# Second MLP: the polynomial's product q(q - 2.5) on ScalarE and GpSimd instead of VectorE

## The reference

```python
def _moe2_ref(x, w_in, w_out) -> np.ndarray:
    h = x @ w_in
    g = h - np.tanh(h)
    return (g @ w_out).astype(np.float32)
```

## Time and profile before

| | |
|---|---|
| median of 3 runs | 1000.71 us (999.56 to 1003.57) |
| span of the profiled execution | 998.4 us |
| TensorE matmuls busy | 971.2 us, 97% |
| VectorE busy | 647.0 us, 65% |
| GpSimd busy | 405.3 us, 41% |
| ScalarE busy | 389.3 us, 39% |
| mean granted TensorE clock | 0.998 of full speed |

### The profile page before, as it was taken

One profiled execution on the slowest core, in us unless ns is written; L12 is line 12 of the kernel. 1 busy time (PEld: TensorE's weight loads), 2 busy tenths in 40 slices (PEclk: granted clock), 3 DMA queues, 4 the chain that ended last, 5 costly groups with the idle time before them and its releaser, 6 DMA issues.

```text
span 998.4 us, 17710 instructions
## 1 busy us (share of the span) xinstructions
PE 971.2 (97%) x6120; PEld 947.5 (95%) x6120; DVE 647.0 (65%) x1136; ACT 389.3 (39%) x790; POOL 405.3 (41%) x398
## 2 busy tenths in 40 slices
PE   8899999999999999999999999999999999999997
PEld 7799999999999999999999889999999999999997
DVE  5954444444444444444446679998999889998886
ACT  4321211211221212112113366665666566666654
POOL 5754453443544444435434553332333233333332
PEclk9999999999999999999999999999999999999999
DMA  8511112021111111120121300000000000000000
GB/s 235 137 25 25 25 25 48 3 48 25 24 25 26 25 24 25 24 48 2 25 83 45 127 1 1 25 1 25 0 24 0 25 0 17 7 9 17 9 17 25
DMA packets 86251, 32.43 MB, mean 32 GB/s; under 512 B 75937, under 2 KB 83106, under 8 KB 86178
## 3 DMA queue, kind: packets, MB, share of 16 engines
q1 hardware_dynamic: 86178, 31.47, 12.3%
HBM read 26.74 MB, written 4.72 MB: 32 GB/s over the span
## 4 chain that ended last, share of the span: by engine, by line
PE 50%; issue 39%; POOL 6%; DVE 2%; POOLq 0%; ACT 0%; DVEq 0%; ACTq 0%
PE bank L634 13%; PE bank L636 12%; PE bank L635 12%; PE bank L709 4%; POOL g_l L409 4%; PE bank L692 2%; PE bank L705 2%; PE bank L701 2%; POOL wout_l L367 1%; PE bank L673 1%; PE bank L679 1%; POOL g_l L359 1%; PE bank L715 1%; DVE win_l L922 1%; POOL wout_l L417 0%
## 5 line engine op out<-in xcount | busy, mean ns | idle before, releaser
L634 PE MATMUL bank<-x_h,win_h 128*128 128x384 f32 x768 | 258.0, 336 | 7.4 <-DVE g_f L910 4.5
L636 PE MATMUL bank<-x_h,win_l 128*128 128x384 f32 x768 | 257.6, 335 | 0.0
L635 PE MATMUL bank<-x_l,win_h 128*128 128x384 f32 x768 | 257.2, 335 | 0.0
L409 POOL TENSOR_TENSOR g_l<-g_f,g_h 128x384 fp32r<-128x384 f32 x128 | 129.9, 1015 | 280.9 <-ACT g_h L513 280.9
L475 ACT ACTIVATE g_h<-g_f 128x384 fp32r<-128x384 f32 x128 | 67.2, 525 | 425.7 <-DVE g_f L910 425.7
L359 POOL TENSOR_TENSOR g_l<-g_f,g_h 128x384 fp32r<-128x384 f32 x128 | 132.0, 1032 | 245.9 <-ACT g_h L475 238.7
L908 DVE TENSOR_SCALAR g_f<-bank 128x384 f32<-128x384 f32 x128 | 71.3, 557 | 201.3 <-PE bank L636 199.3
L634 PEld LDWEIGHTS bank<-x_h,win_h 128*128 128x128 f32 x768 | 144.6, 188 | 9.4 <-DVE g_f L910 6.4
L635 PEld LDWEIGHTS bank<-x_l,win_h 128*128 128x128 f32 x768 | 144.7, 188 | 0.0
L636 PEld LDWEIGHTS bank<-x_h,win_l 128*128 128x128 f32 x768 | 144.7, 188 | 0.0
L967 DVE SCALAR_TENSOR_TENSOR area<-area 128x384 f32<-128x384 f32 x128 | 121.9, 952 | 35.1 <-ACT area L494 32.6
(11 more groups left out here) (99 smaller groups left out, 1396.7 us busy)
## 6 DMA issues: line engine op xcount, KB each, us to landing
out<-area SPq DMA_DIRECT2D x24, 192.0 KB, 1.9
x2T<-in_r SPq DMA_DIRECT2D x23, 192.0 KB, 2.8
x2T<-in_k SPq DMA_DIRECT2D x23, 192.0 KB, 3.4
x2T<-in_v SPq DMA_DIRECT2D x23, 192.0 KB, 3.5
x2T<-in_moe_w_in SPq DMA_DIRECT2D x4, 768.0 KB, 6.5
x2T<-in_moe_w_out SPq DMA_DIRECT2D x4, 768.0 KB, 6.0
area<-in_moe_w_in SPq DMA_DIRECT2D x4, 768.0 KB, 4.3
area<-in_moe_w_out SPq DMA_DIRECT2D x4, 768.0 KB, 4.5
```

The lines of the kernel that those rows point to most:

```text
L409: pool.tensor_tensor(g_l[:, m0 % 4, :], g_f[:, m0 % 2, :], g_h[:, m0 % 4, :].bitcast(F32), ALU.subtract).then_inc(s_gl2, 1)
L634: pe.matmul(dst, wh, xh, start=first, stop=False)
L635: pe.matmul(dst, wh, xl, start=False, stop=False)
L636: return pe.matmul(dst, wl, xh, start=False, stop=last)
```

## The change

ScalarE makes q - 2.5 (new function shifted), GpSimd multiplies it by q (new function square_poly), and VectorE's poly is gone. The compare takes poly's place in VectorE's step; it has moved from ahead of the product of m0 - 1 to behind it, and belongs to slot m0 now. On ScalarE make_ratio moves to the end of the step, behind hi2 of the slot before. On GpSimd square_poly of slot m0 + 1 stands ahead of lo2 of slot m0. The new semaphore s_qq goes from ScalarE to GpSimd; s_pp is now given by GpSimd.

```diff
+            def square_poly(b, m0):
+                m = SLOTS * b + m0
+                pool.wait_ge(s_qq, m + 1)
+                pool.tensor_tensor(ratio[m0 % 2], ratio[m0 % 2], sq[m0 % 2], ALU.mult).then_inc(s_pp, 1)
+
             PEELED = Q
+            square_poly(0, 0)
             for m0 in range(PEELED):
+                square_poly(0, m0 + 1)
                 lo2(0, m0)
...
             with pool.Fori(0, BODIES - 1) as b:
                 for n in range(SLOTS):
+                    square_poly(b, n + PEELED + 1)
                     lo2(b, n + PEELED)
             for n in range(SLOTS - PEELED):
+                if n + PEELED + 1 < SLOTS:
+                    square_poly(LAST, n + PEELED + 1)
                 lo2(LAST, n + PEELED)
...
+            def shifted(b, m0):
+                m = SLOTS * b + m0
+                act.wait_ge(s_sq, m + 1)
+                if is_due(m - 1):
+                    act.wait_ge(s_small, m - 1)
+                act.activation(ratio[m0 % 2], sq[m0 % 2], ACT.Copy, bias=C3_OVER_C5).then_inc(s_qq, 1)
...
                 if m0 < SLOTS or b is not LAST:
                     square(b, m0)
+                    shifted(b, m0)
                     if ends is not None:
                         keep_out(b, ends, 0)
-                    make_ratio(b, m0)
                     table_tanh(b, m0)
                     if ends is not None:
                         keep_out(b, ends, 2)
                 if is_due(SLOTS * b + m0):
                     hi2(b, m0 - 1)
+                if m0 < SLOTS or b is not LAST:
+                    make_ratio(b, m0)
...
             def small_tanh(b, m0):
 
                 m = SLOTS * b + m0
-                dve.wait_ge(s_sq, m + 1)
-                dve.tensor_scalar(is_big[m0 % 2], sq[m0 % 2], Q_SMALL, None, ALU.is_ge).then_inc(s_big, 1)
                 dve.wait_ge(s_ratio, m + 1)
...
-            def poly(b, m0):
+            def find_big(b, m0):
 
                 m = SLOTS * b + m0
                 dve.wait_ge(s_sq, m + 1)
-                dve.scalar_tensor_tensor(out=ratio[m0 % 2], in0=sq[m0 % 2], scalar=C3_OVER_C5, in1=sq[m0 % 2],
-                                         op0=ALU.add, op1=ALU.mult).then_inc(s_pp, 1)
+                dve.tensor_scalar(is_big[m0 % 2], sq[m0 % 2], Q_SMALL, None, ALU.is_ge).then_inc(s_big, 1)
...
                 if m0 < SLOTS or b is not LAST:
-                    poly(b, m0)
+                    find_big(b, m0)
                 if before:
                     act2(b, m0 - 1)
```

## The result

The changed kernel takes 1011.78 us (median of four runs, 1011.28 to 1014.63), the kernel before 1001.56 us when run beside it. The ratio is 1.0112, 95% interval 1.0091 to 1.0133: the change makes the kernel slower by 1.1%. The forecast was 1007.5 us, 6.8 us more than before, with 996 to 1014 us as its range; measured are 10.2 us between the medians and 11.1 us between the spans of the two profiled executions, 1009.5 and 998.4 us. The profiled execution after took 1011.28 us, 1.8 more than its span; the forecast had added 2.3 to the span of before, so some 0.5 of that is scatter between runs, if the two kernels are alike in this.

A forecast was written before the change was run, and what follows sets the result against it. A 3.17 us ring through GpSimd, VectorE and ScalarE, just slower than TensorE's 3.12, was taken to set the loop bodies' time. Terms 4.3 + 1.0 - 1.0 + 2.5 = +6.8 on 1000.71 gave 1007.5 us, range 996 to 1014.

The forecast's parts named there:

- The new ring: Second MLP, ScalarE and VectorE: ratio, product, compare, select, subtraction, g_h, next ratio; 3.22 us a slot in place of 3.17.
- the two terms, 4.3 and 1.0: Three loop bodies: the slower ring adds 4.3 us on some 94 slots, 18 x_h split slots add 1.0.
- the block ends: Accumulator copies at block ends delay g_h by some 0.16 us, as before the change: 0 added.
- Rivals 1 and 2: Ring 3.12, TensorE sets the pace, 998.5 us (0.17); ring 3.18 to 3.20, cheap first slots, about 1003 us (0.15).
- Passes the delay on: Last body of the second MLP: runs at TensorE's pace in both kernels and hands on the delay gained earlier.
- The first slots: Slots with weight pieces on GpSimd: lo comes later and the compare may wait; +2.5 us, 0.5 as other end.
- The loop ends: VectorE's loop end, twice: 1.4 to 2.0 us of the 2.20 gap counts, where about 2.2 did; -1.0 for both.
- upper end: Loop ends: the 2.0 of 1.4 to 2.0 us allows for ScalarE's longer loop body getting such a gap too.
- The third rival: Compare issued 0.2 us late waits out GpSimd's product: +1.1 in each of 124 slots, some 1137 us; chance 0.08.
- Worth, alone: at most 0.05 a slot: Polynomial leaving VectorE breaks the old ring through GpSimd; gain at most 0.05 us a slot, since TensorE stands right behind.
- rival 1: Product to compare costs 0.64 us, so the ring is 3.12 and TensorE sets the pace: 998.5 us; chance 0.17.

The follow-up runs named there:

- The two shifted kernels: The changed kernel with 4, then 8, one-column VectorE memsets ahead of the second MLP's loop, so its code lies later: 1010.29 us and 1013.64 us.
- the first experiment: The changed kernel with the compare of slot m-1 again ahead of the product of m-1, and a VectorE memset taking the select's waits: 989.90 us, ratio 0.9881.

## Why the prediction was right, and where it was not

**The bound and the ring: right.** The new ring was forecast at 3.22 from six terms and is 3.22; none of them is off by more than 0.02 (0.54 for 0.56, 0.75 for 0.74, 0.28 for 0.27, 0.62 for 0.63, 0.60 for 0.59, 0.43). Together the 88 steps of the table give +5.39, where the two terms, 4.3 and 1.0, said 5.3. That this fits so well is in part luck: at 0.051 a step the ring makes 4.5, the splits add 0.5 and not 1.0 (the slots are 3.25 to 3.26), and the block ends, forecast at 0, add 0.3. (32 x 3.17 is 101.4 and not 101.5; nothing rests on it.) Rivals 1 and 2 fell: the 0.19 of the wait for the product stands ahead of the compare as it stood ahead of the polynomial.

**The last body: right for TensorE's steps, not for what the delay does.** They are 3.12 in both kernels. But the end hangs on g_l, whose ring goes on at 3.17 in the kernel before and at 3.12 in the kernel after, and whose last step is 0.83 longer after. "Passes the delay on" left both out; they nearly cancel (-0.61 and +0.83).

**The first slots: right, and from the upper end.** The compare took 1.04, 1.07 and 1.08 us beside the weight pieces; the three steps of g_l are 3.94 to 4.02, where they were 3.17 to 3.27. +2.30 were measured and +2.5 forecast. The Trainium skill's rule ("SBUF — State Buffer", section "Who interferes with whom"), that a VectorE instruction in a two-port mode waits out a GpSimd instruction that came first, is the one the trace bears out here: 1.07 from SBUF, 0.56 from PSUM, both issued 0.15 behind GpSimd.

**The loop ends: the step that failed.** "*Loop end of VectorE* ... **-1.0** for both." The two steps across the branch gave -0.38: a part of the gap is hidden, but less. Over the ring's own step the gap costs 1.83 and 1.88 us now (steps of 5.05 and 5.10) and cost 2.09 before (5.26), where the prediction had 1.4 to 2.0 and about 2.2. The "upper end" of that sentence also came about. ScalarE now has such a gap (2.0 us, twice, in the waits above, none before); it overlaps VectorE's 2.3 and so costs little: the next compare, which needs its square, comes 0.86 behind the product and not 0.75. The Trainium skill ("Runtime: NRT & Kernel Launch", section "Instruction fetch mechanics") says that a taken branch whose target lies outside the fetched window stalls; the trace agrees as far as it goes, since ScalarE's loop body has 328 instructions in the trace now and had 264, when no gap stood there. No run here changes the length alone.

**What was missing: the compare of slots 34, 66 and 98, +3.35, and its consequence, +0.70.** The third rival said what happens when the compare is 0.2 late, priced it at +1.1 a slot (measured 1.12), and named the margin, 0.2. It was given 0.08, because "ring and product both hang on the same ratio, so the order is the same in every slot". This is the sentence that failed. The order is the same only while VectorE issues at once, and in three slots it does not. The two shifted kernels show that this is a matter of where the code lies. The +0.70 from slot 98 to 99 is TensorE's stop and its half clock; with the long compare gone, 0.75 of that step goes too. The rest of the last body, +0.16 in all, is its own (above).

**The sum again**, with what was measured: -0.43 before the first slot, 2.30, 5.39, -0.38, 3.35 and 0.86 in the last body make 11.09. To the forecast's 6.8 the last two add 4.21, the loop ends 0.62 and the ring with its splits 0.09; 0.43 before the first slot and 0.20 in the first slots go off again. So over a third of the measured delay is in no term of the forecast. The range, which was not drawn for these, took it in; that the time lies within it is luck to that extent, the direction and the ring are not.

**"Worth, alone: at most 0.05 a slot": wrong, though it did not enter the sum.** Without the polynomial's wait the kernel is 14 us faster, three times the 4.7 that 0.05 on 94 slots makes. One slot was compared with one slot. A ring that is clearly faster than TensorE (2.63 us there, 2.89 in the first experiment, which gains 0.23 a slot) builds up time in hand, and block ends and splits are paid from that. A ring level with TensorE, as in rival 1, would build up nothing; no run shows that case. So the change had more to win than the prediction saw, and the first experiment is what it is worth with the compare outside the ring.

**VectorE's busy time** fell by 92 us, forecast was "about the polynomial's 122". The group of the polynomial held 121.9 us. Back come 6.4 in the compares (44.9 to 51.3 in all) and some 3 in instructions that are now beside more GpSimd work. The last 20 or so are in how busy time is counted (the durations alone fall by 112.7): back to back, one record begins 0.08 to 0.09 before the one ahead of it ends (the product at 704.59 and the compare until 704.67), such time counts once, and the new order has fewer such pairs.

## What to carry to other kernels

When work moves off an engine, write down the new ring, and also in which order the engines reach a shared resource and with what margin: a margin of 0.2 us is not safe where an issue delay of 0.36 us exists. Put an instruction that can be held up by another engine outside the ring (a slot earlier or later), or let it start while that engine is idle; here the order (with the memset) was worth 9 us without the split, and with it decided between 1.1% slower and 1.2% faster. And compare a ring's pace with the bounding engine's over a whole block, not a slot: what it gains there also pays for the stops.

## What the runs showed of the hardware

- VectorE loses 0.36 us at a fixed place of its code, with no other engine as the cause. Eight more one-column instructions ahead of the loop moved it by one slot. The Trainium skill ("Runtime: NRT & Kernel Launch", section "Instruction fetch mechanics") calls the crossing into the next block mostly hidden; if it is this, it is not hidden here (0.55 in place of 0.19 between product and compare).
- A compare from SBUF to SBUF takes 0.36 us, and 0.89 to 1.20 when it is issued early in a GpSimd instruction; late in one it takes less (0.42 when it begins 0.2 before GpSimd's end, in the first experiment). From PSUM it takes 0.56 in both cases. A copy with predicate whose data is in PSUM (0.57 to 0.60) and a product with one input in PSUM (0.55) keep their times beside GpSimd.
- The wait for GpSimd is in the recorded duration and not in the start: the compare at 691.88 is recorded as running while GpSimd's product does. The idle time of 0.55 ahead of it holds the 0.36 of lateness and nothing of this wait.
- After a stop of 2.04 us TensorE ran ten matmuls at 0.32 us with a granted clock of 0.52; after two stops of 2.01 us in the same kernel the granted clock stayed at 1.00.
